# The last tile of layer 1 as one block of 128 rows, the tile before it as a whole tile

## The reference

```python
def _moe2_ref(x, w_gate, w_output_gate, w1, w2):        # N, D, E, F = 14336, 192, 8, 1024
    e_idx = np.argmax(x @ w_gate, axis=1)
    ...                                                 # probs: softmax of the logits; gate_w: the chosen one
    eom = 1.0 / (1.0 + np.exp(-(x @ w_output_gate)))
    for e in range(E):
        mask = e_idx == e
        h = np.maximum(x[mask] @ w1[e], 0.0)
        ye = h @ w2[e]
        out[mask] = gate_w[mask, None] * eom[mask, e, None] * ye
```

## Time and profile before

| | |
|---|---|
| median of 3 runs | 1282.5 us (1275.85 to 1284.53) |
| profiled execution | 1281.93 us, span 1280.4 us |
| mean granted TensorE clock | 0.946 |
| busy: PE, DVE, ACT, POOL | 91%, 67%, 48%, 34% of the span |
| layer 1 | from about 790 us to the end |

### The profile page before, as it was taken

One profiled execution on the slowest core, in us unless ns is written; L12 is line 12 of the kernel. 1 busy time (PEld: TensorE's weight loads), 2 busy tenths in 40 slices (PEclk: granted clock), 3 DMA queues, 4 the chain that ended last, 5 costly groups with the idle time before them and its releaser, 6 DMA issues.

```text
span 1280.4 us, 38886 instructions
## 1 busy us (share of the span) xinstructions
PE 1161.9 (91%) x13470; PEld 1054.3 (82%) x13470; DVE 855.9 (67%) x2335; ACT 615.3 (48%) x1083; POOL 436.3 (34%) x478
## 2 busy tenths in 40 slices
PE   2578774999889999999999999999999999999996
PEld 2567763888779888889999989888999998999996
DVE  2899997879889999997777787733333443334332
ACT  1777775345456555554545445333333333333332
POOL 1077786633323433432222222322222221222222
PEclk9776685999999999999999999999999999999999
DMA  8588966799997799566443426476424546424451
GB/s 222 176 279 283 296 216 201 177 204 232 255 289 172 189 288 280 144 207 168 107 112 94 119 67 153 94 193 179 117 57 113 165 112 167 114 55 109 112 136 56
DMA packets 236048, 214.78 MB, mean 168 GB/s; under 512 B 176895, under 2 KB 209307, under 8 KB 229954
## 3 DMA queue, kind: packets, MB, share of 16 engines
q1 hardware_dynamic: 209408, 148.85, 44.7%
q0 software_dynamic: 25520, 64.49, 17.1%
q10 hardware_dynamic: 1042, 0.47, 0.2%
HBM read 114.22 MB, written 69.62 MB: 144 GB/s over the span
## 4 chain that ended last, share of the span: by engine, by line
PE 56%; DVE 22%; issue 7%; DMA 6%; SPq 4%; ACT 3%; DVEq 0%; POOL 0%; ACTq 0%; POOLq 0%
PE bank L871 55%; DVE am L1136 3%; DVE hl L1367 2%; DMA wslot<-image 2%; DVE split L1211 2%; PE bank L876 1%; DMA stage<-in_moe_w 1%; SPq L426 1%; DVE split L1214 1%; DVE wslot L1238 1%; DVE wam L1100 1%; DVE wam L1098 1%; SPq L427 1%; DVE xsl L1140 1%; ACT rowt L727 1%
## 5 line engine op out<-in xcount | busy, mean ns | idle before, releaser
L1367 DVE SCALAR_TENSOR_TENSOR hl<-bank,hh 128x512 f16<-128x512 f32 x480 | 331.1, 690 | 336.3 <-ACT hh L812 330.4
L812 ACT ACTIVATE hh<-bank 128x512 f16<-128x512 f32 x480 | 286.3, 596 | 461.3 <-PE bank L871 452.1
L871 PE MATMUL bank<-xT,wslot 128*128 128x256 f16 (+1 forms) x3920 | 467.3, 274 | 13.4 <-DMA xT<-rows 7.5
L871 PE MATMUL bank<-wslot,hh 128*128 128x192 f16 x3136 | 421.5, 247 | 8.5 <-DVE hl L1367 4.9
L871 PEld LDWEIGHTS bank<-xT,wslot 128*128 128x128 f16 (+1 forms) x3920 | 328.7, 98 | 70.9 <-issue 22.3
L871 PE MATMUL bank<-wslot,hl 128*128 128x192 f16 x1568 | 386.3, 246 | 0.0
L871 PEld LDWEIGHTS bank<-wslot,hh 128*128 128x128 f16 x3136 | 279.4, 98 | 28.6 <-issue 13.5
L699 POOL DMA_INDIRECT out_tokens<-y,idxt x120 | 116.7, 972 | 364.7 <-ACT y L824 311.4
L640 POOL DMA_INDIRECT rows<-rowt,idxp x120 | 126.4, 1053 | 321.5 <-PE bank L871 196.7
L871 PEld LDWEIGHTS bank<-wslot,hl 128*128 128x128 f16 x1568 | 153.6, 98 | 0.1
L615 POOL DMA_INDIRECT rows<-rowab,idxa x96 | 107.4, 1119 | 55.1 <-issue 39.7
(11 more groups left out here) (175 smaller groups left out, 1270.8 us busy)
## 6 DMA issues: line engine op xcount, KB each, us to landing
wslot<-image SPq DMA_DIRECT2D x21, 1024.0 KB
split<-image SPq DMA_DIRECT2D x16, 1024.0 KB
wslot<-image SPq DMA_DIRECT2D x21, 768.0 KB, 5.2
split<-image SPq DMA_DIRECT2D x16, 768.0 KB, 4.9
image<-split POOLq DMA_DIRECT2D x18, 512.0 KB
image<-split SPq DMA_DIRECT2D x8, 1024.0 KB, 4.2
image<-split POOLq DMA_DIRECT2D x9, 768.0 KB
stage<-in_moe_w SPq DMA_DIRECT2D x8, 768.0 KB, 9.8
```

Source lines behind the costliest of these rows:

```text
L812: nc.scalar.activation(hh[:, c, :], bank[c][:, :], ACT.Relu).then_inc(hh_out, 1)
L871: return nc.tensor.matmul(o, a, b_, start=start, stop=stop, skip_group_check=True)
L1367: V.scalar_tensor_tensor(hl[:, c, :], bank[c][:, :], 0.0, hh[:, c, :], ALU.max, ALU.subtract).then_inc(hl_out, 1)
```

## The change

The last tile of layer 1 (119) has one block of 128 rows, in slot 2. Tile 118, until now mixed, is a whole tile in slot 0 and takes entry 13; so odd tiles from 73 to 117 take the entries 14 to 36, one higher each. The block numbered 21, which no input needs, is gone. Relu, subtraction, contraction, outputs, token index and scatter of tile 119 work on 128 rows. In SP the quad of tiles 112 to 115 is now straight code as well, in POOL the quad of tiles 116 to 119. The diff, without what only renames (`slots` to `parts`, a list of start row, rows and slot):

```diff
@@ -271,7 +271,7 @@
 
         def one(body, g):
 
-            body(g, g // 2, g % 2, g // 2 % 2, g // 4, False, layer_of(g, 0), g // 4 % QUADS >= MIXQ)
+            body(g, g // 2, g % 2, g // 2 % 2, g // 4, False, layer_of(g, 0), g < GT - 4 and g // 4 % QUADS >= MIXQ)
 
         def quad(body, i, prep, l, mix):
 
@@ -297,12 +297,18 @@
             for g in TAIL:
                 one(body, g)
 
+        def half_tile(g):
+
+            return isinstance(g, int) and g == GT - 1
+
         def two_blocks(s, v, mix):
 
             return mix and v == 1 and s == 0
 
         def blocks_upto(s, v, i, l, mix):
 
+            if isinstance(i, int) and i == 2 * QUADS - 1:
+                return 2 * MIXED - 1
             if not mix:
                 return l * MIXED
             return i - (1 + l) * MIXQ + v
@@ -311,7 +317,11 @@
 
             if s:
                 return k + 1
-            return i + 1 + (1 + l) * MIXQ if mix else k + 1 - l * MIXED
+            return i + 1 + (1 + l) * MIXQ if mix else k + 1 - blocks_upto(s, 0, i, l, mix)
+
+        def rows_of(g, a):
+
+            return a.rearrange("p (u r) -> p u r", u=2)[:, :, 0:P] if half_tile(g) else a
 
         def routes(g, s, l):
 
@@ -430,8 +440,11 @@
             def load_x(g, x, l):
                 load_rows(tab[0:1, 1, bass.ds(g, 1)], 0, T, x, l, x_loaded[x], meta_loaded[x])
 
+            def load_block(i, x, l):
+                load_rows(blk[0:1, 1, 0, bass.ds(i, 1)], 0, P, x, l, x_loaded[x], meta_loaded[x])
+
             def load_blocks(i, x, l):
-                load_rows(blk[0:1, 1, 0, bass.ds(i, 1)], 0, P, x, l, x_loaded[x], meta_loaded[x])
+                load_block(i, x, l)
                 load_rows(blk[0:1, 1, 1, bass.ds(i, 1)], 1, P, x, l, x2_loaded, meta2_loaded)
 
             def expert(g):
@@ -470,7 +483,7 @@
                 if late(g, 1):
                     sp.wait_ge(h_done, g * NP)
                     sp.sem_inc(store_turn, 1)
-                    if last + 1 < GT and not (mix and c == 1):
+                    if last + 2 < GT and not (mix and c == 1):
                         needs.append((None if other else change(g + 1), lambda: expert(g + 1), ahead, 1 - s))
                 for need in needs:
                     load_next(*need, 0)
@@ -479,11 +492,13 @@
                         sp.wait_ge(meta_out, g)
                     if mix and c == 0:
                         load_blocks(i, 2, l)
+                    elif half_tile(g + 2):
+                        load_block(i, 3, l)
                     else:
                         load_x(g + 2, (c + 2) % XS, layer_of(g + 2, l))
                 if first:
                     load_w_part(block_expert(i + 2, v), l, 2 + v, s)
-                for a in range(2 if again else 0):
+                for a in range((1 if half_tile(last + 4) else 2) if again else 0):
                     needs.append((block_change(i + 1, a), lambda a=a: block_expert(i + 1, a), l, 2 + a))
                     load_next(*needs[-1], 0)
                 if needs:
@@ -549,9 +564,9 @@
             for g in range(NT + 4 * MIXQ - 8, NT + 4 * MIXQ):
                 one(loads, g)
             sp.wait_ge(pads_stored, 32 * E)
-            with sp.Fori(QUADS + MIXQ, 2 * QUADS - 1) as i:
+            with sp.Fori(QUADS + MIXQ, 2 * QUADS - 2) as i:
                 quad(loads, i, False, 1, True)
-            for g in range(GT - 4, GT):
+            for g in range(GT - 8, GT):
                 one(loads, g)
 
 
@@ -578,13 +593,16 @@
             def numbers(dst, n, step, base):
                 return nc.gpsimd.iota(dst, [[step, n]], base=base, channel_multiplier=0, allow_small_or_imprecise_dtypes=True)
 
-            for g0, n, tail in [(l * NT + g, n, tail) for l in range(2) for g, n, tail in ((0, EARLY[l], 0), (EARLY[l], 4 * MIXQ - EARLY[l], MIXED))]:
-                even, odd = n // 2 + tail, n // 2
+            for l, g0, n, tail in [(l, l * NT + g, n, tail) for l in range(2) for g, n, tail in ((0, EARLY[l], 0), (EARLY[l], 4 * MIXQ - EARLY[l], MIXED))]:
+                extra = l if tail else 0
+                even, odd = n // 2 + tail + extra, n // 2
                 if n:
                     numbers(tidx[:, g0:g0 + n:2], n // 2, 1, 0)
                     numbers(tidx[:, g0 + 1:g0 + n:2], n // 2, 1, even)
                 for c in range(4 if tail else 0):
-                    numbers(tidx[:, g0 + n + c:g0 + n + 4 * tail:4], tail, 2 if c % 2 else 1, even + odd + c // 2 if c % 2 else n // 2)
+                    m = tail - extra if c == 2 else tail
+                    numbers(tidx[:, g0 + n + c:g0 + n + 4 * m:4], m, 2 if c % 2 else 1, even + odd + c // 2 if c % 2 else n // 2)
+            numbers(tidx[:, GT - 2:GT - 1], 1, 1, (4 * MIXQ - EARLY[1]) // 2 + MIXED)
             numbers(bidx[:, :], 2 * MIXED, 1, 0)
             for t_, pat, b0, cm in ((desc, [[-1, E]], E, 0), (eidx, [[1, E]], 0, 0),
                                     (base0, [[CAP, E]], 0, 0), (ids, [[WIN, G]], WIN - 1, -1)):
@@ -695,7 +713,7 @@
                 pool.wait_ge(token_ready, g - NT + 1)
                 pool.wait_ge(y_out, g + 1)
                 pool.sem_inc(pool_turn, 1)
-                for j in range(J):
+                for j in range(1 if half_tile(g) else J):
                     nc.gpsimd.indirect_dma_start(
                         out[:, :], bass.IndirectOffsetOnAxis(idxt[:, s, j:j + 1], 0),
                         y[:, s, j, :], None, bounds_check=N - 1, oob_is_err=False).then_inc(scat_t[s], 16)
@@ -713,12 +731,14 @@
             scatter_row(PAIRS - 1, 1, 3)
             for g in range(NT + 3, NT + 8):
                 one(scatter, g)
-            with pool.Fori(QUADS + 2, 2 * QUADS) as i:
+            with pool.Fori(QUADS + 2, 2 * QUADS - 1) as i:
                 quad(scatter, i, False, 1, False)
+            for g in TAIL:
+                one(scatter, g)
             for v in range(2):
                 pool.wait_ge(scat_p[v], 16 * W2T * (PAIRS // 2))
             for s in range(2):
-                pool.wait_ge(scat_t[s], 16 * J * (NT // 2))
+                pool.wait_ge(scat_t[s], 16 * (J * (NT // 2) - s))
 
 
         @block.scalar
@@ -820,7 +840,7 @@
                         act.wait_ge(scat_t[s], (k - FIRST) * 16 * J)
                     else:
                         act.wait_ge(xs_ready, STEPS + k)
-                for j in range(J):
+                for j in range(1 if half_tile(t) else J):
                     last = nc.scalar.activation(y[:, s, j, :], bank[YB + s][:, j * D:(j + 1) * D], ACT.Identity, scale=tf[:, s, j:j + 1])
                 last.then_inc(y_out, 1)
 
...
+            def parts_of(t, s, v, mix):
+
+                if half_tile(t):
+                    return ((0, P, 2),)
+                return ((0, P, 2), (P, P, 3)) if two_blocks(s, v, mix) else ((0, T, s),)
...
+                    for j, slot in [(j, slot) for p0, n, slot in parts for j in range(p0 // P, (p0 + n) // P)]:
...
-                contract(GT - 1, 1, (1, 1), c)
+                contract(GT - 1, 1, parts_of(GT - 1, 1, 1, False), c)
...
-                V.scalar_tensor_tensor(hl[:, c, :], bank[c][:, :], 0.0, hh[:, c, :], ALU.max, ALU.subtract).then_inc(hl_out, 1)
+                V.scalar_tensor_tensor(rows_of(t, hl[:, c, :]), rows_of(t, bank[c][:, :]), 0.0, rows_of(t, hh[:, c, :]),
+                                       ALU.max, ALU.subtract).then_inc(hl_out, 1)
```

## The result

| | kernel before | changed kernel |
|---|---|---|
| median, device time, 14 runs each in turn | 1279.28 us (1269.77 to 1284.55) | 1285.06 us (1279.52 to 1291.76) |
| ratio, 95% interval | | 1.0052, 1.003 to 1.0073 |
| profiled execution | 1281.93 us, span 1280.4 us | 1284.73 us, span 1283.2 us |
| mean granted TensorE clock | 0.946 | 0.944 |

The forecast was 1277.2 us; the range (1272.0 to 1282.5) doesn't hold the result.

The account below looks back on a forecast made before the run. TensorE was taken to bound the kernel. Tile 119 -3.8, the end -3.6 and tile order +2.1 gave -5.3 us against 1281.93: 1276.6, stated as 1277.2 us because the median ran 0.6 higher; range 1272.0 to 1282.5.

Parts of the forecast that it names:

- What bounds the kernel: Second layer: almost only TensorE; a mixed tile costs what a whole one does, 8.17 against 8.13 us.
- Tile 118 as a whole tile: Tile 118, whole instead of two blocks: 8.13 us against 8.17, so nothing gained or lost.
- Tile 119, -3.8: Last tile, first hidden matmul to last matmul: 7.4 us with one block instead of 11.24, 3.8 saved.
- Order of whole tiles, +2.1: Weight waits at tiles 85 and 109 add 4.6 us, the wait of tile 117 goes (2.5): +2.1 us.
- rival 2: Waits at tiles 85 and 109 bring TensorE's clock down, each costing 1.7 us more: 1280.6 us, chance 0.17.
- Rivals 1, 5 and 6: Inherited waits don't come: 1272.6, chance 0.13; narrow matmuls or last chunks paced elsewhere: 1278.2, 0.07; tail not cut: 1280.9, 0.05.
- Rival 3: Slower than before: weight part 1 lands late in tiles 85 and 109, at 7.0 us giving 1285.8; chance 0.07.
- The end, -3.6: After the last matmul: one activation fewer, no second scatter, 4.4 us to the end instead of 8.0, 3.6 saved.
- Rival 4: At the end, the 2 us between the last two scatters come ahead of the only scatter: 1279.2 us, chance 0.08.
- The prediction's own sign of being wrong: At the end: the forecast is wrong if more than 5 us follow the last matmul.

Follow-up runs that it names:

- e3: Changed kernel with tile 118 taking the last entry, 36, instead of 13, so odd tiles keep their earlier entries; ratio to the kernel before 1.0022.
- e7: Kernel before with straight POOL code for tiles 116 to 119 and without tile 118's second scatter (padding alone); ratio to the kernel before 1.0063.
- f1: Changed kernel, still straight code, with two scatters in tile 119, the second rewriting tile 117's block; ratio to the kernel before 1.0004.
- f3: Changed kernel with one more scatter of 128 rows, to a spare array, behind tile 119's only one; ratio to the kernel before 0.9975.
- g1: e3 with one extra scatter, to a spare array, just ahead of tile 118's; ratio to the kernel before 0.9939.
- e1: Kernel before with POOL's scatters of tiles 116 to 119 as straight code behind its loop; ratio to the kernel before 1.0019.

## Why the prediction was wrong, step by step

- **What bounds the kernel:** right. Tile 118 as a whole tile cost nothing (7.57 between its first relu and tile 119's, 8.17 before, and the 0.6 is tile 119's narrower chunk 0).
- **Tile 119, -3.8:** measured -3.9. Eight narrow matmuls go by in 0.45 us, 0.056 each (1263.83 to 1264.28). The relu took 0.38, the subtraction 0.42 (0.45 and 0.42 taken). The 81 ns of "TensorE: Matmul & The Clock Gate" in the Trainium skill (section "Back-to-back issue gap") didn't show: the trace has 56.
- **Order of whole tiles, +2.1:** measured 2.36 + 2.15 - 2.72 = +1.8 in the profiled execution, +2.1 over all kernels (worked out beside e3). The size is right, the place by half: I had the whole wait at part 1, but the late part 0 took 1.0 and 0.5 of it. Part 1 went out at 984.48 (985.5 forecast). There are seven loads in place of six, and tile 115's caused no wait.
- **The clock (rival 2):** stayed at 2.4 GHz. Each wait was split in two of at most 1.30 us, shorter than the 2.33 after which it had stayed up in the earlier trace rows. Rivals 1, 5 and 6 didn't come either. Rival 3 has the right sign, slower, for a wrong reason: part 1 landed 4.6 us after its issue at tile 85 and not 7.
- **The end, -3.6: the failing step.** "The end comes 3.1 after that" was carried over from the earlier trace rows. It was 12.1 after the last scatter: 2.4 of landing, 0.2, the DRAIN's 9.3, 0.2. In place of -3.6 the end gave +5.9. The prediction's own sign of being wrong, more than 5 us behind the last matmul, came: 13.9 behind its end. Up to the landing the end was cut by 3.15 (scatter 2.0 after the last matmul's start, 5.15 before): the 0.4 short of the forecast is the queue behind tile 118's second scatter.
- **Rival 4** asked where the 2 us before the last scatter go. That was the right thing to doubt, "for a reason the trace doesn't show", and its alternatives were the wrong ones: the pause before the scatter, or gone. It went, and 9 us came in its place. Nothing on the page of before priced this; line L88 of before, which the prediction doesn't use, has only a DRAIN of 0.225 us. The pause had no releaser, and I took it to go away with the instruction that it stood before. e7, f1 and f3 show that the long DRAIN comes when that instruction goes and leaves when another one takes its place.
- But for the DRAIN the forecast's sum is about right: -5.3 + 9.1 = +3.8 against 1281.9, where the profiled execution has +2.8, or +3.5 without the 0.75 by which it was ahead at tile 84.

## What to carry to other kernels

Read the closing instructions of every engine with the chain: a span can end in a GpSimd DRAIN that no busy column shows. Where GpSimd issues scatters up to the end, a version with one scatter more or fewer there is worth a run; here one more took 0.83% off e3 (g1), and 0.77% off the changed kernel (f3). And where a pause in a queue has no row that explains it, don't assume that it only disappears with the instruction next to it: give a chance to the case that its work turns up elsewhere, at another price.

## What was not expected of the hardware

- GpSimd's closing DRAIN took 0.225, 0.387, 0.632, 3.245, 5.205, 8.472, 9.288, 9.302 or 9.432 us, and the same to the nanosecond in many kernels (9.288 in five, 0.225 in seven).
- A scatter that writes no row shortens the time by being there: ratios of 1.0019 with it (e1) and 1.0063 without (e7), 8.2 and 15.6 us from the last matmul's start to the end.
- Idle time in an early tile is split between the two parts of a weight load; the sum (2.36 and 2.15 us, 2.3 forecast) could be worked out from the queue, the split was not.
